# Rotary attention and two feed-forward layers on one core: tile 25's scaling, the values' rounding and a bank rule where the layers begin

## The reference

```python
q_rot, k_rot = rotate(q), rotate(k)              # rotary embedding, halves of 32
scores = matmul(q_rot, k_rot.T) / sqrt(64)
attn = exp(scores - max(scores)); attn = attn / (sum(attn) + 1e-9)
x = (attn @ v) as 1152 tokens x 512
h = x @ w_in;  x = (h * sigmoid(h)) @ w_out      # 512 -> 2048 -> 512
h = x @ w_in2; out = elu(h) @ w_out2             # 512 -> 2048 -> 512
```

## Time and profile before

| | |
|---|---|
| median of 3 runs | 550.04 us (549.96 to 550.08) |
| profiled execution | 550.01 us |
| its span, first to last instruction | 548.2 us |
| mean granted TensorE clock | 1.00 |
| PE busy | 536.9 us, 98% |
| ACT busy | 380.6 us, 69% |
| POOL busy | 345.7 us, 63% |
| DVE busy | 290.8 us, 53% |
| chain that ended last | PE 90%, ACT 4%, DMA 2% |

### The profile page before, as it was taken

The page is one execution under the profiler, slowest core; times in us unless marked ns, Lnnn a source line. Parts: engine busy times, 40 slices in busy tenths (PEclk is TensorE's granted clock), DMA queues, the critical chain, the costliest instruction groups (busy, mean ns, idle before and its releaser), DMA issues.

```text
span 548.2 us, 9533 instructions
## 1 busy us (share of the span) xinstructions
PE 536.9 (98%) x3259; PEld 525.7 (96%) x3259; DVE 290.8 (53%) x603; ACT 380.6 (69%) x829; POOL 345.7 (63%) x277
## 2 busy tenths in 40 slices
PE   8799999999999999999999999999999999999997
PEld 7688889999999999999999999999999999999997
DVE  5789865744368853537663348784344530067400
ACT  3889889967668977769886668886666653356531
POOL 5988989859746656546655754445455666566662
PEclk9999999999999999999999999999999999999999
DMA  8677665576365456444444333333334444444440
GB/s 320 191 220 200 162 198 149 165 220 183 120 169 158 123 146 182 143 121 137 120 129 132 117 112 105 112 115 120 111 120 128 127 135 122 128 119 132 134 145 29
DMA packets 45790, 79.52 MB, mean 145 GB/s; under 512 B 6832, under 2 KB 14384, under 8 KB 45744
## 3 DMA queue, kind: packets, MB, share of 16 engines
q1 hardware_dynamic: 44016, 76.57, 48.0%
q10 hardware_dynamic: 1728, 2.36, 1.2%
HBM read 63.57 MB, written 2.36 MB: 120 GB/s over the span
## 4 chain that ended last, share of the span: by engine, by line
PE 90%; ACT 4%; DMA 2%; issue 1%; SPq 1%; POOL 1%; DVE 1%; ACTq 0%; POOLq 0%
PE banks L1202 72%; PE banks L1095 5%; PE banks L1072 3%; PE banks L1078 3%; PE banks L1163 3%; PE banks L1156 2%; DMA k_raw<-k 1%; ACT prob L572 1%; PE banks L1138 1%; ACT pt L592 1%; PE banks L1116 1%; POOL k_raw L400 0%; DMA k_st<-k_raw 0%; ACT v_st L561 0%; PE banks L1165 0%
## 5 line engine op out<-in xcount | busy, mean ns | idle before, releaser
L450 POOL TENSOR_TENSOR w_lo<-w_raw,w_hi 128x512 fp32r<-128x512 f32 x192 | 247.2, 1292 | 183.5 <-ACT w_hi L649 183.4
L649 ACT CAST w_hi<-w_raw 128x512 fp32r<-128x512 f32 x189 | 117.0, 622 | 31.7 <-PE banks L1202 29.4
L1202 PE MATMUL banks<-x_lo,w_hi 128*128 128x384 f32 x384 | 128.8, 336 | 0.3 <-DVE g_lo L918 0.3
L1202 PE MATMUL banks<-x_hi,w_lo 128*128 128x384 f32 x384 | 128.6, 335 | 0.0
L1202 PE MATMUL banks<-g_hi,w_lo 128*128 128x384 f32 x384 | 128.5, 335 | 0.0
L1202 PE MATMUL banks<-x_hi,w_hi 128*128 128x384 f32 x384 | 128.5, 335 | 0.0
L1202 PE MATMUL banks<-g_lo,w_hi 128*128 128x384 f32 x384 | 128.5, 335 | 0.0
L1202 PE MATMUL banks<-g_hi,w_hi 128*128 128x384 f32 x384 | 128.5, 335 | 0.0
L787 DVE TENSOR_REDUCE neg_max<-banks 128x1 f32<-128x576 f32 x72 | 54.1, 753 | 52.7 <-PE banks L1078 51.4
L661 ACT ACTIVATE act_buf<-banks 128x384 f32<-128x384 f32 x96 | 47.4, 493 | 37.5 <-PE banks L1202 37.0
L1202 PEld LDWEIGHTS banks<-x_lo,w_hi 128*128 128x128 f32 x384 | 72.1, 188 | 1.3 <-issue 1.0
(11 more groups left out here) (119 smaller groups left out, 729.5 us busy)
## 6 DMA issues: line engine op xcount, KB each, us to landing
w_raw<-w SPq DMA_DIRECT2D x192, 256.0 KB, 2.7
q_raw<-q SPq DMA_DIRECT2D x11, 384.0 KB, 3.6
q_one<-q_raw SPq DMA_DIRECT2D x44, 96.0 KB, 2.9
k_raw<-k SPq DMA_DIRECT2D x7, 576.0 KB, 5.5
k_st<-k_raw SPq DMA_DIRECT2D x28, 144.0 KB, 2.9
v_raw<-v SPq DMA_DIRECT2D x8, 320.0 KB, 3.4
out<-act_buf ACTq DMA_DIRECT2D x12, 192.0 KB, 2.5
k_both<-k_st SPq DMA_DIRECT2D x15, 144.0 KB, 3.1
```

The lines of the kernel that those rows point to most:

```text
L450: nc.gpsimd.tensor_tensor(w_st[LO][:, slot, :], w_raw[:, slot, :], w_st[HI][:, slot, :].bitcast(F32), ALU.subtract).then_inc(w_lo_done, 1)
L649: nc.scalar.copy(w_st[HI][:, slot, :], w_raw[:, slot, :]).then_inc(w_hi_done, 1)
L1202: last = nc.tensor.matmul(dst, w_st[wp][:, slot, m * P:(m + 1) * P], src[xp][:, tile, :], start=start and n == 0, stop=stop and n == 2)
```

## The change

The edits, by engine:

- SP: the values of pair 4 are loaded ahead of weight 4 and the placing of head 9, instead of behind weight 6.
- POOL: before the key product of pair 5 a wait until three low parts of the attention output are done (`x_lo_done` at 3; DVE's line 873).
- ACT: the values of pair 4 are rounded at the end of unit 0's place instead of unit 4's. At unit 3's place weight 5 is rounded behind tile 25's exponential, followed at once by tile 25's scaling and weight 6. At unit 4's place the high part of unit 2 comes before the activation of unit 3.
- DVE: at unit 3's place tile 25's maximum comes first, and its inversion before the low part of tile 24. At unit 4's place the low part of unit 2 comes before unit 3's first step.
- PE: use 6 of a chunk waits for use 0's bank instead of use 3's.

```diff
--- before.py
+++ after.py
@@ -344,11 +344,11 @@
                 load_keys(r + 2)
             place(4, 0)
             place_both(H)
+            load_values(4)
             load_unit(RING)
             place(4, 1)
             for n in range(RING + 1, RING + AHEAD):
                 load_unit(n)
-            load_values(4)
             load_queries(6)
             load_keys(6)
             for n in range(ALL_UNITS):
@@ -493,6 +493,8 @@
             for n in range(AHEAD):
                 weight_lo(n)
             rope_queries(5)
+
+            pool.wait_ge(x_lo_done, 3)
             rope_keys(5)
             for n in range(ALL_UNITS):
                 i, j = H + n // 8, n % 8
@@ -732,16 +734,21 @@
                 beside = i < ITERS
                 first = n % UNITS < 8
                 tile = tile_at(i, j) if beside else None
+                if n == 4:
+
+                    evict_b(n - 2)
                 evict_a(n - 1)
-                evict_b(n - 2)
-                if beside and j and tile_at(i, j - 1) is not None and QN * i + tile_at(i, j - 1) + 1 < STEPS:
+                if n != 4:
+                    evict_b(n - 2)
+                if beside and j and n != 4 and tile_at(i, j - 1) is not None \
+                        and QN * i + tile_at(i, j - 1) + 1 < STEPS:
                     scale_tile(QN * i + tile_at(i, j - 1) + 1)
                 if tile is not None:
                     probs_hi(QN * i + tile)
                     if tile in (-1, 2):
                         end_hi(i - 1 if tile < 0 else i)
 
-                if n in (2, 3):
+                if n == 2:
                     weight_hi(n + AHEAD - 1)
                 if n + AHEAD < ALL_UNITS and n not in (1, 2, 3):
                     weight_hi(n + AHEAD)
@@ -750,12 +757,16 @@
                 if tile is not None and QN * i + tile + 1 < STEPS:
                     exp_tile(QN * i + tile + 1)
                 if n == 3:
+                    weight_hi(n + AHEAD - 1)
+                    scale_tile(QN * i + tile + 1)
                     weight_hi(n + AHEAD)
                 if i % H == 0 and i <= ITERS and j == 0:
                     if n == 0:
                         copy_out_lo(i - 1)
                         scale_tile(H * QN)
                     output_hi(p - 1)
+                    if n == 0:
+                        values_hi(4)
                 if not beside:
                     continue
                 if n in (6, 7):
@@ -767,7 +778,7 @@
                 if i % H == H - 1 and j == 7:
                     copy_out_lo(i)
                 if i % 2 == 0:
-                    if j == 4 and p < 8:
+                    if j == 4 and 4 < p < 8:
                         values_hi(p)
                     if j == 7 and not first:
                         output_hi(p - 1)
@@ -991,12 +1002,15 @@
                 beside = i < ITERS
                 first = n % UNITS < 8
                 tile = tile_at(i, j) if beside else None
+
+                if n == 3:
+                    max_tile(QN * i + tile + 1)
+                if n == 4:
+                    evict_lo(n - 2)
                 evict_first(n - 1)
-                if n == 3:
-                    evict_lo(n - 2)
-                if tile is not None and tile >= 0 and QN * i + tile + 1 < STEPS:
+                if n != 3 and tile is not None and tile >= 0 and QN * i + tile + 1 < STEPS:
                     max_tile(QN * i + tile + 1)
-                if n != 3:
+                if n != 4:
                     evict_lo(n - 2)
                 evict_second(n - 1)
                 if i % H == 0 and i <= ITERS and j == 0:
@@ -1010,10 +1024,12 @@
                     end_lo(i - 1)
                     max_tile(QN * i)
                 elif tile is not None:
+                    if n == 3:
+                        invert_tile(QN * i + tile + 1)
                     probs_lo(QN * i + tile)
                     if tile == 2:
                         end_lo(i)
-                if tile is not None and QN * i + tile + 1 < STEPS:
+                if n != 3 and tile is not None and QN * i + tile + 1 < STEPS:
                     invert_tile(QN * i + tile + 1)
                 if not beside:
                     continue
@@ -1178,7 +1194,7 @@
 
             def bank_free(use):
 
-                b = use - 3
+                b = use - (6 if use % USES == 6 else 3)
                 if use == 0 or use == 1:
                     pe.wait_ge(exp_done, H * QN)
                 elif use == 2:
```

## The result

The changed kernel took 548.72 us (median of 14 runs, 548.05 to 549.30), the kernel before 549.98 (14 runs, 549.31 to 550.80). The ratio is 0.9978, with a 95% interval of 0.9971 to 0.9985: 1.2 us or 0.22% less. In a later set of runs it was 0.9983 (0.9975 to 0.9992). So the difference is on the line of 0.2% on which the forecast put it, and the median lies inside the range of 548.6 to 549.5.

A forecast was written before the change was run, and what follows sets the result against it. PE, busy for 98% of the span, was taken to bound the kernel; of 1.35 in its two gaps ACT's queue lets 1.09 through: 550.01 - 1.09 = 548.92, plus 0.03 for the median, 548.95; range 548.6 to 549.5.

The forecast's parts named there:

- the line of 0.2%: A difference of 0.2% (1.10 us) is what a measurement can tell from no change; the forecast gain was 1.09.
- The two gaps of 0.83 and 0.52: PE standing still in chunk 0: 0.83 around tile 25's transposes before unit 5, 0.52 before unit 6's second matmul; together 1.35.
- 1.09: ACT's gain before unit 4's activation, 0.63 + 0.46, passed on to unit 7's low part and unit 10: the kernel's gain.
- The chances, 0.41 and 0.51: Whole kernel: chance 0.41 of measuring faster and 0.51 of measuring the same, with 0.08 for slower.
- The wait that was to come next: PE before unit 10 waits for DVE's low part of unit 7: there at about 91.95, it may start at 92.33.
- The values: ACT's rounding of unit 4's values, 0.63, moves behind unit 0's last output rounding, into idle time of 1.75 before 71.54.
- the third rival: Tile 25's exponential does not follow its maximum; only the values' rounding, 0.63, is gained: 549.4. Chance 0.07.
- Unit 4 and unit 7: Small margins on PE: unit 4 has 0.06 and unit 7 0.1 us to spare.
- POOL's wait: The key product, held until DVE's subtraction ends, takes 2.67 instead of 3.20; all behind it on POOL moves by 0.19.
- The slower rival: Values land late and hold ACT before unit 0's activation, one for one after about 70.9; landing at 74.0 gives 552.05. Chance 0.08.
- the first gap: PE from unit 4's last matmul to unit 5's first, tile 25's transposes waiting for ACT's scaling: 1.98 instead of 1.15, costing 0.83.

The follow-up runs named there:

- the late load: The changed kernel with the values' load left behind weight 6 on SP, against the kernel before: median 550.14 us, ratio 1.0007; profiled in two executions.
- the latest load: The changed kernel with the values' load moved behind the loads of queries 6 and keys 6, against the kernel before: median 554.15 us, ratio 1.0081.
- the next change: The changed kernel with the rounding of keys 6 moved one unit later in ACT's queue, against the kernel before: median 548.38 us, ratio 0.9975.

## Why the prediction was right

- **Where the time stood.** The two gaps of 0.83 and 0.52 are gone in the changed kernel, as said, and the kernel does not get their sum. The step on which the forecast rested, that ACT's queue and not PE's gaps sets unit 10, was tested from both sides: the bank rule alone gives 0.00, tile 25's order alone 0.42 of its 0.83, and 0.57 less of ACT's work ahead of unit 7's low part gives 0.3 more.
- **The size.** 1.09 was forecast, and the stretch gives 1.05 and 1.02. Of the first profile's missing 0.04, most lies between the exponential and the scaling: 75.83 - 74.48 = 1.35, where I had 76.08 - 74.78 = 1.30; the exponential itself took 0.78 here (0.74 before). Forecast 548.95, measured 548.72: by the medians the change gained 1.26, about 0.2 more than the stretch gives. In the later set of runs it was 0.85, about 0.2 less. So the 0.2 either way is the spread of the times, and that the first median came out below the forecast is chance. The chances, 0.41 and 0.51 for either side of the 0.2%, fit a ratio that came out at 0.9978 and 0.9983.
- **The wait that was to come next.** Unit 10's restart was put at 92.33. It is 92.10, which with a head shorter by 0.27 is 92.37, and its second matmul is 0.25 behind. The wait is 0.39 against 0.16 before.
- **The values.** Said to fit into the idle time; it does: ACT still idles 1.10 before 71.25. But the third rival's price, 0.63 for the values' rounding alone, was too high: that kernel gained 0.40.
- **Unit 4 and unit 7** had 0.06 and 0.1 to spare. Both show a step of 0.20 to 0.22 at the second matmul instead of 0.17: 0.03 to 0.05 each, covered by unit 10.
- **POOL's wait** was to move the rest of POOL by 0.19, by the reading that the product of 3.20 already stood behind DVE. The reading holds in the main (3.16 without the wait, 2.68 with it). The size was a little off: the key sum stands 69.30 - 67.32 = 1.98 behind the head's end, where it was 69.31 - 67.59 = 1.72, so 0.26; the pads still came in time. The Trainium skill ("SBUF — State Buffer", the section on the two sides) says that whoever starts first keeps the port pair. The runs agree that one of the two loses nearly the other's length, but in all six profiles without the wait POOL was first by the recorded starts, by 0.07 to 0.11, and it was POOL that lost (3.14 to 3.20). So the recorded starts don't tell who wins when they lie this close; what does, no run here shows.
- **The slower rival** did not happen, but its mechanism is real: one for one from about 71 on, as the two executions with the late load show. What the forecast missed is that a wait can cost more than itself, through PE's clock: with the values at 7.12 behind the head's end one for one gives a stretch of 24.74 + 7.12 - 3.32 = 28.54 (24.74 is the forecast's stretch, 3.32 the point up to which ACT's idle time takes the wait, 70.91 - 67.59), and 29.79 was measured. And when the load is not moved along, landings of 3.8 to 5.2 after the issue are enough to be late: the load's move on SP is the part of the change that makes the values' rounding safe.
- **What I had wrong in the experiments.** The values alone were to give 0.6 and gave 0.40. I had followed ACT's queue and left PE out: with the first gap still there, unit 5's end at 81.63 holds the activation that ACT could have started near 81.45. The reorderings are therefore worth more together (1.05) than one by one (0.82). For the latest load I had left out the clock.

Left open: whether POOL's wait protects DVE in some executions, and why the first loads land up to 0.8 apart, which accounts for most of the head's 0.9. In the first execution with the late load the head, 67.81, also had a stretch of lower clock in it (see the last section).

## What to carry to other kernels

A gap on the busiest engine is worth its length only if whatever feeds the next few steps gets sooner too. Follow the feeding queue to its next idle time; the gain is at most the smaller of the two. Undo the parts one by one before you credit one of them: here one part was worth nothing, and worth 0.24 after the next change. And work that you move to the head of an in-order queue takes its transfer's landing with it, so move the load with it and look at the spread of the times, not only at one profile.

## What I had not expected of the hardware

- The landing of one and the same load, at the same place in SP's order, took 3.8 us in one execution and 5.2 in another, and the stretch followed, 24.98 and 26.07. The kernel's time ranged from 548.5 to 551.3 over 12 runs.
- A PE wait of 3.52 was followed by 3.2 us at a granted clock of 0.51, and one of 1.0 by none. The Trainium skill ("TensorE: Matmul & The Clock Gate", Part 1) says that PE falls to the lower level after idling; these two waits agree with that. The length of the last wait alone does not decide it: in the first execution with the late load the clock was at 0.50 from 15 to 17 us, after waits of 0.53 (before 8.63) and 1.58 (before 14.10), while in the kernel before a wait of 1.60 at the same place, with none at 8.6, left it at 1.00.
- In chunk 0, where POOL's product was well under way, DVE's subtraction with two SBUF inputs took 1.14 and 1.28 instead of 0.54 in the kernel before (at 37.73 and 50.63, about 1.9 us into the product); at 66 us, where both started within 0.11, DVE took 0.54 and POOL was the longer one, in every profile in which no wait parted them.
